# Linear attention on one core: the state product as four 64x64 parts, key sums on GpSimd, and a new order of the unit's work

## The chip, the cores and the metric

The kernel runs on one core of one Trainium2 chip. The metric is device time in microseconds (us) of one launch; less is better. Before the change it is 872.39 us (median of 3 runs, 872.06 to 872.72).

## What is computed

Three layers follow one another: linear attention, a feed-forward layer with a mixing over tokens, and a mixture of experts. The change touches the first one alone. Its reference, for batch 4, 8 heads, sequence 576, head dimension 64 and 128 features:

```
def phi(x):
    proj = np.einsum('bhsd,df->bhsf', x, w_phi)
    proj = proj - np.max(np.abs(proj), axis=-1, keepdims=True)
    return np.concatenate([np.exp(proj), np.exp(-proj)], axis=-1)
q_p, k_p = (phi(q), phi(k))
kv = np.einsum('bhsf,bhsd->bhfd', k_p, v)
z = np.sum(k_p, axis=2)
num = np.einsum('bhsf,bhfd->bhsd', q_p, kv)
den = np.einsum('bhsf,bhf->bhs', q_p, z)[..., None] + 1e-06
return (num / den).astype(np.float32)
```

`kv` is the state, `z` are the key sums. Afterwards `u = x + (x.T @ U @ V).T` (the mixing, with factors U and V of rank 32), a hidden layer of 2048, and the experts.

## The kernel before

**Units.** Two (batch, head) pairs make a unit; partitions 0 to 63 hold one pair, 64 to 127 the other ("halves"). There are 16 units of 9 token tiles of 64 rows (T = 9). The attention is a pipeline of 18 steps: in step s, PE (TensorE) works on the newest unit s (transposes of raw q and k, `transposes`), on the newer unit s-1 (projection by w_phi, `project`) and on the older unit s-2 (the turned queries `turn_q`, the state product `state`, the output product `output`). Steps 0 to 3 and 16, 17 are written out, steps 4 to 15 run in a loop of two steps. Every engine has its own in-order list of work; semaphores join them.

**The engines of one step.** DVE (VectorE) reads each projection from PSUM twice, for the greatest absolute value (L1014) and to subtract it (L1022), in three groups per unit, and divides the output of an earlier unit (`divide`, L1030 to L1037). ACT (ScalarE) copies the transposed q and k out of PSUM (`evac_T`, L840), makes exp(x) and exp(-x) of the turned queries (`exp_q`, L845, L846) and of the keys (`exp_k`, L853, L854), and copies the finished state out (`evac_kv`, L861). The work on transposes, turned queries and keys is cut in three groups of three tiles (NG, GT).

**The state product before.** For each of the 9 tiles, each sign of the exponent and each half, one matmul (L1533) has 128 features of `kp` as its stationary operand and 65 columns of `vv` moving: 64 of v and a column of ones, which gives the key sum with the state. The 36 matmuls of a unit are spread over the step between transposes and turns, cut by the constant LATE. The state comes out with features on partitions, which is how the output product (L1549) wants it.

**GpSimd before.** POOL splits the weights of the feed-forward layer into a high and a low part (`split_piece`, L677 and L680), one piece for two steps of attention, as they arrive by DMA. When the pieces of the first matrix are done, it makes the factor V ready in both parts (`spread_v`, L716 to L728), and raises the semaphore uv_ready up to 8. Behind that it waits for the last output product (n_done) and splits the second matrix.

**The end of the attention.** In step 16 PE has, behind the output product of unit 14, the product of the rows by U (job "odd", L1671, 18 matmuls of 64 rows by 64 columns with 512 moving columns). In step 17 it has, ahead of the output product of unit 15, the three "mix" jobs of the first block (L1685, L1686), which read what `spread_v` makes:

```
                    if c == 0:
                        pe.wait_ge(uv_ready, 8)
```

Then come the transposes "uT" of the first block and the feed-forward layer.

## Time and profile before

| | us |
|---|---|
| median of 3 runs | 872.39 |
| the profiled execution's own time | 872.83 |
| its span | 870.7 |
| PE busy | 857.1 |
| DVE busy | 402.4 |
| ACT busy | 342.1 |
| POOL busy | 153.6 |

The span is the time from the first to the last instruction in the trace; the execution's own time is 2.1 us longer. Busy time of PE counts records of matmuls, which overlap in its pipeline, so that it says when PE had work and not how well it was used. A matmul in fp32 leaves two records in the trace: "x72" are 36 matmuls. A start in the timeline, less the start of the row ahead of it on the same engine, is what that row's work took of the engine.

### The profile page before, as it was taken

How to read it: one execution, taken by the hardware profiler on the slowest of the kernel's cores; microseconds unless marked ns; L12 is line 12 of the kernel's file. 1: busy time of each engine (PE TensorE's matmuls, PEld its weight loads, DVE VectorE, ACT ScalarE, POOL GpSimd, SP SyncE). 2: the span in 40 equal slices, each digit the busy share in tenths (PEclk: the TensorE clock that was granted, in tenths of full speed). 3: DMA queues.
4: the chain of work that ended last, by engine and by line, in shares of the span. 5: the costliest groups of instructions: out<-in, count | busy, mean ns of one | idle time of the engine just before them, and what ended most of it. 6: DMA issues, size and time to landing. Idle time of an engine off the chain costs nothing.

```text
span 870.7 us, 19055 instructions
## 1 busy us (share of the span) xinstructions
PE 857.1 (98%) x6984; PEld 749.7 (86%) x6985; DVE 402.4 (46%) x732; ACT 342.1 (39%) x767; POOL 153.6 (18%) x158
## 2 busy tenths in 40 slices
PE   7999999999999999999999999999999999999996
PEld 6999999789899899799989889998778888888885
DVE  4676776531245335425635663552773342432221
ACT  3677666521136326414612531541332342432221
POOL 0311222476000000000000000029152121212111
PEclk9999999999999999999999999999999999999999
DMA  6644442227522102102101210513431341311111
GB/s 139 160 116 126 130 117 78 65 92 55 1 73 61 37 37 61 49 0 71 63 13 49 59 39 37 193 49 134 156 127 69 134 148 36 126 48 42 36 36 42
DMA packets 52469, 67.65 MB, mean 78 GB/s; under 512 B 29768, under 2 KB 29896, under 8 KB 52424
## 3 DMA queue, kind: packets, MB, share of 16 engines
q1 hardware_dynamic: 42552, 44.90, 19.7%
q10 hardware_dynamic: 6512, 11.64, 4.4%
q0 software_dynamic: 3360, 10.49, 3.7%
q8 instruction: 31, 0.51, 0.3%
q14 instruction: 14, 0.11, 0.0%
HBM read 57.58 MB, written 9.98 MB: 78 GB/s over the span
## 4 chain that ended last, share of the span: by engine, by line
PE 93%; DVE 3%; ACT 1%; issue 1%; DMA 0%; POOLq 0%; SPq 0%; DVEq 0%; ACTq 0%
PE bank L1619 23%; PE bank L1621 23%; PE bank L1620 23%; PE bank L1533 8%; PE bank L1549 4%; PE bank L1506 4%; PE bank L1808 2%; PE bank L1494 1%; PE bank L1517 1%; PE bank L1671 1%; PE bank L1760 1%; PE bank L1690 1%; DVE stage L1094 1%; ACT stage L916 1%; PE bank L1685 1%
## 5 line engine op out<-in xcount | busy, mean ns | idle before, releaser
L1063 DVE SCALAR_TENSOR_TENSOR hid_lo<-bank,hid_hi 128x384 fp32r<-128x384 f32 x96 | 53.5, 558 | 211.1 <-ACT hid_hi L892 211.1
L1619 PE MATMUL bank<-uT_hi,W 128*128 128x384 f32 x384 | 129.4, 337 | 0.3 <-DVE uT_lo L1082 0.3
L1621 PE MATMUL bank<-uT_hi,W 128*128 128x384 f32 x384 | 129.6, 337 | 0.0
L1620 PE MATMUL bank<-uT_lo,W 128*128 128x384 f32 x384 | 128.9, 336 | 0.0
L892 ACT ACTIVATE hid_hi<-bank 128x384 fp32r<-128x384 f32 x96 | 46.9, 488 | 185.5 <-PE bank L1621 185.3
L916 ACT ACTIVATE stage<-stage 128x512 f32<-128x512 f32 x135 | 84.6, 627 | 78.6 <-DVE stage L1094 72.1
L1619 PE MATMUL bank<-W,hid_hi 128*128 128x512 f32 x288 | 114.1, 396 | 0.7 <-DVE hid_lo L1063 0.7
L1621 PE MATMUL bank<-W,hid_lo 128*128 128x512 f32 x288 | 113.7, 395 | 0.0
L1620 PE MATMUL bank<-W,hid_hi 128*128 128x512 f32 x288 | 113.4, 394 | 0.0
L1094 DVE TENSOR_TENSOR stage<-rows,stage 128x512 f32<-128x512 f32 x135 | 89.0, 687 | 9.8 <-ACT stage L916 8.5
L1325 DVE TENSOR_TENSOR hT_lo<-bank,hT_hi 128x512 fp32r<-128x512 f32 x40 | 27.7, 691 | 105.5 <-ACT hT_hi L953 105.5
L1619 PEld LDWEIGHTS bank<-uT_hi,W 128*128 128x128 f32 x384 | 72.2, 188 | 4.3 <-DVE uT_lo L1082 0.5
L1533 PE MATMUL bank<-vv,kp 64*128 64x65 f32 x1152 | 75.3, 273 | 0.0
L1620 PEld LDWEIGHTS bank<-uT_lo,W 128*128 128x128 f32 x384 | 72.1, 188 | 3.8
L947 ACT ACTIVATE hrow<-bank 128x512 f32<-128x512 f32 x40 | 23.9, 599 | 125.7 <-PE bank L1621 125.7
L1621 PEld LDWEIGHTS bank<-uT_hi,W 128*128 128x128 f32 x384 | 72.0, 188 | 0.0
L1533 PEld LDWEIGHTS bank<-vv,kp 64*128 64x128 f32 x1152 | 69.8, 188 | 2.0 <-issue 0.8
L1619 PE MATMUL bank<-W,xT_hi 128*128 (+1 forms) x160 | 64.9, 405 | 0.3 <-DVE xT_lo L1320 0.2
L1619 PEld LDWEIGHTS bank<-W,hid_hi 128*128 128x128 f32 x288 | 54.1, 188 | 12.7 <-issue 1.8
L1619 PE MATMUL bank<-W,hT_hi 128*128 (+1 forms) x160 | 64.2, 401 | 0.0
L1621 PEld LDWEIGHTS bank<-W,hid_lo 128*128 128x128 f32 x288 | 54.0, 188 | 11.7
L1014 DVE TENSOR_REDUCE top<-bank 128x6 f32<-128x768 f32 x48 | 45.7, 952 | 37.3 <-PE bank L1506 37.3
(274 smaller groups left out, 1430.4 us busy)
## 6 DMA issues: line engine op xcount, KB each, us to landing
rows<-in_moe_w SPq DMA_DIRECT2D x12, 1024.0 KB, 6.4
stage<-gate_rows ACTq DMA_DIRECT2D x38, 256.0 KB, 3.2
stage<-in_moe_w_ch SPq DMA_DIRECT2D x16, 512.0 KB, 3.9
qk_raw<-in_q SPq DMA_DIRECT2D x32, 144.0 KB, 2.9
vv<-in_v SPq DMA_DIRECT2D x32, 144.0 KB, 3.2
x_rows<-rows SPq DMA_DIRECT2D x6, 768.0 KB, 3.2
qk_raw<-in_k SPq DMA_DIRECT2D x30, 144.0 KB, 2.9
late_stage<-in_moe_w SPq DMA_DIRECT2D x4, 1024.0 KB, 6.0
```

The source lines that it names most:

```text
L892: act.activation(hid_hi[:, n % 2], bank[:, HB[n % 2], 0:TOK], ACT.Relu).then_inc(hid_hi_out, 1)
L916: act.activation(product(m), product(m), ACT.Copy, accum_out=logits[:, b * BLK + i, g:g + 1])\
L1014: dve.tensor_reduce(most, src, AX.X, ALU.max, apply_absolute_value=True).then_inc(top_done, 1)
L1063: dve.scalar_tensor_tensor(out=hid_lo[:, n % 2], in0=bank[:, HB[n % 2], 0:TOK], scalar=0.0, in1=hid_hi[:, n % 2].bitcast(F32), op0=ALU.max ...
L1094: dve.tensor_tensor(product(m), rows[:, b * BLK + i, :], gate_row(k), ALU.mult)\
L1325: dve.tensor_tensor(hT_lo[:, 4 * g:4 * g + 4], bank[:, 2 + g, :].rearrange("p (c n) -> p c n", c=4), hT_hi[:, 4 * g:4 * g + 4].bitcast(F32 ...
L1506: mm = pe.matmul(bank[:, pair + a, t * NF:t * NF + NF], qkT[rr, g, t, :], wphi[rr, :], start=True, stop=True)
L1533: mm = pe.matmul(bank[:, KV_BANK + half, sign * VW:(sign + 1) * VW], kp[par][rr, t // GT, t % GT, sign, :], vv[par][rr, t, :], start=(t == ...
L1549: mm = pe.matmul(dst[rr, t, :], qpT[:, n // GT, sign, n % GT, rr], kv[:, half, VW * sign:VW * sign + VW], start=(sign == 0), stop=(sign == 1))
L1619: pe.matmul(dst, lhs_hi, rhs_hi, start=start, stop=False)
L1620: pe.matmul(dst, lhs_hi, rhs_lo, start=False, stop=False)
L1621: return pe.matmul(dst, lhs_lo, rhs_hi, start=False, stop=stop)
```

## The change

- **State product.** `vv` becomes the stationary operand (64 rows, 64 columns) and `kp` the moving one (128 columns). The two signs go to the two halves of the output partitions, the two halves of the rows to two PSUM banks: four products on four quarters of the array. All 36 matmuls stand in one piece. The state now comes out with the features along the free dimension, and has no key sums.
- **Turning back.** `evac_kv_raw` copies the state to SBUF, `turn_kv` transposes it with four matmuls, and `evac_kv` copies it out again, now in two instructions.
- **Key sums.** `sum_keys` on POOL adds the nine tiles of `kp` in four additions: two of 768 elements per partition and two of 256. Four matmuls of one moving column (in `turn_kv`) then add over the partitions.
- **Groups.** Raw q and k are transposed in two groups, of 4 and 5 pairs of tiles, and the queries turned in two, of 5 and 4 tiles; projection and key exponentials stay in three.
- **Order.** PE and ACT have a new order within a step; on ACT the three `exp_k` of a unit now stand together at the end of the step. On POOL `sum_keys` stands ahead of each piece of weights, and ahead of `spread_v`.
- The column of ones in `vv`, and its two memsets on DVE, go.

The diff, cut:

```diff
+    TT = (4, T - 4)
+    NT = len(TT)
     OT = (5, T - 5)
...
+        K_TURNED = slice(NF, NF + 2 * D)
+        K_SUMS = slice(NF + 2 * D, NF + 2 * D + 2)
...
+            def sum_keys(u, par):
+                if not (isinstance(u, int) and u == 0):
+                    pool.wait_ge(k_summed, u)
+                pool.wait_ge(kp_done, NG * u + 2)
+                settled(pool)
+                pool.tensor_tensor(k_part[:, :, :, :], kp[par][:, 0], kp[par][:, 1], ALU.add).then_inc(k_step, 1)
+                pool.wait_ge(k_step, NG * u + 1)
+                pool.wait_ge(kp_done, NG * u + 3)
+                settled(pool)
+                pool.tensor_tensor(k_part[:, :, :, :], k_part[:, :, :, :], kp[par][:, 2], ALU.add).then_inc(k_step, 1)
+                pool.wait_ge(k_step, NG * u + 2)
+                settled(pool)
+                pool.tensor_tensor(k_part[:, 0], k_part[:, 0], k_part[:, 1], ALU.add).then_inc(k_step, 1)
+                pool.wait_ge(k_step, NG * u + 3)
+                if not (isinstance(u, int) and u < 2):
+                    pool.wait_ge(kv_turned, u - 1)
+                settled(pool)
+                pool.tensor_tensor(k_sum[par][:, :, :], k_part[:, 0], k_part[:, 2], ALU.add).then_inc(k_summed, 1)
...
             with pool.Fori(1, UNITS // 4) as n:
                 for i in range(2):
+                    sum_keys(4 * n + 2 * i, 0)
+                    sum_keys(4 * n + 2 * i + 1, 1)
                     split_piece(2 * n + i, i, 0, (2 * n + i) * WCH)
             spread_v()
...
                 def exp_k(u, p, g):
                     act.wait_ge(p_out, NG * u + (2, 3, 3)[g])
                     if not (isinstance(u, int) and u < 2):
                         act.wait_ge(kv_done, u - 1)
+                        act.wait_ge(k_summed, u - 1)
...
+                def evac_kv_raw():
+                    act.wait_ge(kv_done, s - 1)
+                    act.activation(kv_raw[:, :, :], bank[:, KV_BANK:KV_BANK + 2, 0:NF], ACT.Copy).then_inc(kv_raw_out, 1)
+
                 def evac_kv():
                     u = s - 2
-                    act.wait_ge(kv_done, u + 1)
+                    act.wait_ge(kv_turned, u + 1)
                     if not (isinstance(u, int) and u == 0):
                         act.wait_ge(n_done, OUTS * u)
-                    act.activation(kv[:, :, :], bank[:, KV_BANK:KV_BANK + 2, 0:2 * VW], ACT.Copy)\
-                       .then_inc(kv_out, 1)
+                    act.activation(kv.rearrange("p h s n -> p s h n")[:, :, :, 0:D],
+                                   bank[:, KV_BANK:KV_BANK + 2, K_TURNED].rearrange("p s (h n) -> p s h n", n=D), ACT.Copy)
+                    act.activation(kv[:, :, :, D], bank[:, KV_BANK:KV_BANK + 2, K_SUMS], ACT.Copy).then_inc(kv_out, 1)
...
+                def state():
                     u = s - 2
+                    pe.wait_ge(v_loaded[par], 32 * (u // 2) + 32)
+                    if not (isinstance(u, int) and u == 0):
+                        pe.wait_ge(n_out, OUTS * u)
+                    for t in range(T):
+                        if t in (0, 2 * GT):
+                            pe.wait_ge(kp_done, NG * u + 2 + t // (2 * GT))
+                            settled(pe)
+                        for sign, cols in enumerate(HALVES):
+                            for half, rr in enumerate(HALVES):
+                                mm = pe.matmul(bank[cols, KV_BANK + half, 0:NF], vv[par][rr, t, :],
+                                               kp[par][rr, t // GT, t % GT, sign, :], start=(t == 0), stop=(t == T - 1))
+                    mm.then_inc(kv_done, 1)
+
+                def turn_kv():
+                    u = s - 2
+                    pe.wait_ge(kv_raw_out, u + 1)
+                    settled(pe)
+                    for half in range(2):
+                        for sign, rr in enumerate(HALVES):
+                            pe.transpose(bank[:, KV_BANK + sign, NF + D * half:NF + D * half + D], kv_raw[rr, half, :],
+                                         ident[rr, rr])
+                    pe.wait_ge(k_summed, u + 1)
+                    settled(pe)
+                    for sign in range(2):
                         for half, rr in enumerate(HALVES):
+                            mm = pe.matmul(bank[:, KV_BANK + half, K_SUMS.start + sign:K_SUMS.start + sign + 1],
+                                           k_sum[par][rr, sign, :], ones[rr, 0:1], start=True, stop=True)
+                    mm.then_inc(kv_turned, 1)
```

**Where PE's work moved.** PE, one full step (step 3) before. The names: `qk_raw` raw q and k, `proj` projected queries being turned, `kp` with `vv` the state, `kv` with `qpT` the output.

```order
L1494 MATMUL bank<-ident,qk_raw 128x64 x6
L1506 MATMUL bank<-wphi,qkT 128x128 x12
L1517 MATMUL bank<-ident,proj 128x64 x6
L1533 MATMUL bank<-vv,kp 128x65 x12
L1494 MATMUL bank<-ident,qk_raw 128x64 x6
L1533 MATMUL bank<-vv,kp 128x65 x10
L1517 MATMUL bank<-ident,proj 128x64 x6
L1533 MATMUL bank<-vv,kp 128x65 x12
L1494 MATMUL bank<-ident,qk_raw 128x64 x6
L1533 MATMUL bank<-vv,kp 128x65 x2
L1506 MATMUL bank<-wphi,qkT 128x128 x6
L1517 MATMUL bank<-ident,proj 128x64 x6
```

PE, the same step of the change, with the output product that ends it (before, too, 36 of them ended the step).

```order
L1550 MATMUL bank<-ident,proj 128x64 x10
L1540 MATMUL bank<-wphi,qkT 128x128 x12
L1528 MATMUL bank<-ident,qk_raw 128x64 x8
L1565 MATMUL bank<-kp,vv 64x128 x36
L1550 MATMUL bank<-ident,proj 128x64 x8
L1540 MATMUL bank<-wphi,qkT 128x128 x6
L1575 MATMUL bank<-ident,kv_raw 128x64 x4
L1581 MATMUL bank<-ones,k_sum 128x1 x4
L1528 MATMUL bank<-ident,qk_raw 128x64 x10
L1595 MATMUL bank<-kv,qpT 64x65 x36
```

The state is one piece of 36 in place of four, six groups of transposes are four, and turning the state back and the key sums stand between the last projection and the output.

**Where GpSimd's work moved.** POOL, from the end of the loop over the pieces of the first matrix, before:

```order
L677 COPY W<-stage 128x1024
L678 REGISTER_ALU
L680 ISA
L680 TENSOR_TENSOR W<-stage,W 128x1024
L734 REGISTER_ALU
L734 COMPARE_AND_BRANCH
L716 MEMSET v_pair 128x1152
L721 COPY v_pair<-v_raw 32x9x64 x4
L724 CAST v_hl<-v_pair 128x1152
L728 TENSOR_TENSOR v_hl<-v_pair,v_hl 32x1152 x2
```

POOL in the change, from the last half of that loop's body (in its last round: the additions of unit 15, the last piece) to the same place:

```order
L749 TENSOR_TENSOR k_part<-kp 128x768
L750 REGISTER_ALU
L751 REGISTER_ALU
L753 TENSOR_TENSOR k_part<-k_part,kp 128x768
L756 TENSOR_TENSOR k_part<-k_part 128x256
L761 TENSOR_TENSOR k_sum<-k_part 128x256
L686 ISA
L689 ISA
L689 COPY W<-stage 128x1024
L690 REGISTER_ALU
L692 ISA
L692 TENSOR_TENSOR W<-stage,W 128x1024
L767 REGISTER_ALU
L767 COMPARE_AND_BRANCH
L728 MEMSET v_pair 128x1152
```

Four additions per unit now stand ahead of the pieces, and the work of `spread_v`, in its old place behind the loop, stands behind the additions of the last unit.

**ACT in one step of the change:** queries, transposes, the raw state, queries, the turned state, transposes, and then all keys of the newer unit.

```order
L881 ACTIVATE qpT<-bank 128x640
L882 ACTIVATE qpT<-bank 128x640
L875 ACTIVATE qkT<-bank 128x512
L895 ACTIVATE kv_raw<-bank 128x256
L881 ACTIVATE qpT<-bank 128x512
L882 ACTIVATE qpT<-bank 128x512
L902 ACTIVATE kv<-bank 128x2x2x64
L904 ACTIVATE kv<-bank 128x4
L875 ACTIVATE qkT<-bank 128x640
L890 ACTIVATE kp<-proj 128x3x128
L891 ACTIVATE kp<-proj 128x3x128
```

Before, the first group of keys stood at the end of a step, and the other two at the head of the next one, around a copy of transposes.

## Rows read from the trace of the kernel before

**Rows 1.** Page, part 1 (busy time) and part 4 (shares of the chain).

```profile
PE 857.1 (98%) x6984; PEld 749.7 (86%) x6985; DVE 402.4 (46%) x732; ACT 342.1 (39%) x767; POOL 153.6 (18%) x158
PE 93%; DVE 3%; ACT 1%; issue 1%; DMA 0%; POOLq 0%; SPq 0%; DVEq 0%; ACTq 0%
```

**Rows 2.** Busy time by stretch: attention (stretch, length, busy PE, PEld, DVE, ACT, POOL, clock, DMA).

```profile
98.10:157.80 59.70, 59.70 (x1318) 58.38 (x1316) 42.16 (x69) 41.20 (x97) 17.01 (x12) 1.00 0.41 109
```

**Rows 3.** Timeline of PE, one step (start, us, engine, line).

```profile
102.92 2.32 PE L1549 MATMUL bank<-kv,qpT 128*64 128x65 f32 x72
105.17 0.40 PE L1494 MATMUL bank<-ident,qk_raw 64*128 64x64 f32 x6
105.41 1.56 PE L1506 MATMUL bank<-wphi,qkT 64*128 64x128 f32 x24
106.80 0.34 PE L1517 MATMUL bank<-ident,proj 64*128 64x64 f32 x6
107.11 1.56 PE L1533 MATMUL bank<-vv,kp 64*128 64x65 f32 x24
108.50 0.35 PE L1494 MATMUL bank<-ident,qk_raw 64*128 64x64 f32 x6
108.69 1.28 PE L1533 MATMUL bank<-vv,kp 64*128 64x65 f32 x20
...
112.47 0.34 PE L1517 MATMUL bank<-ident,proj 64*128 64x64 f32 x6
112.74 2.32 PE L1549 MATMUL bank<-kv,qpT 128*64 128x65 f32 x72
```

**Rows 4.** Timeline of PE at the end of attention (steps 16 and 17).

```profile
161.28 2.32 PE L1549 MATMUL bank<-kv,qpT 128*64 128x65 f32 x72
163.53 4.51 PE L1671 MATMUL bank<-rows,u_pair 64*64 64x512 f32 x36
167.97 0.40 PE L1517 MATMUL bank<-ident,proj 64*128 64x64 f32 x6
...
169.64 1.08 PE L1678 MATMUL bank<-z_odd,ident 128*64 128x512 f32 x4
170.65 1.33 PE L1533 MATMUL bank<-vv,kp 64*128 64x65 f32 x20
...
174.35 0.50 PE L1685 MATMUL bank<-z_hi,v_hl 128*128 128x512 f32 x1
```

**Rows 5.** Timeline of ACT behind an output product's start.

```profile
103.79 0.53 ACT L853 ACTIVATE kp<-proj 128x384 f32<-128x384 f32 x1
104.20 0.53 ACT L854 ACTIVATE kp<-proj 128x384 f32<-128x384 f32 x1
```

**Rows 6.** Group of instructions of ACT (busy, mean ns, idle before).

```profile
L947 ACT ACTIVATE hrow<-bank 128x512 f32<-128x512 f32 x40 | 23.9, 599 | 125.7 <-PE bank L1621 125.7
```

**Rows 7.** Groups of instructions of POOL.

```profile
L680 POOL TENSOR_TENSOR W<-stage,W 128x1024 fp32r<-128x1024 f32 x10 | 24.0, 2398 | 1.8 <-POOL W L677 1.8
L680 POOL TENSOR_TENSOR W<-stage,W 128x1024 f32 x6 | 14.1, 2356 | 1.6 <-POOL W L677 1.6
L785 POOL TENSOR_TENSOR W<-rows,W 128x2048 fp32r<-128x2048 f32 x3 | 13.8, 4615 | 0.2
```

**Rows 8.** Timeline of POOL, the last piece and the preparation of V.

```profile
148.30 2.35 POOL L680 TENSOR_TENSOR W<-stage,W 128x1024 f32 x1 [0.26 <-POOL W L677]
150.59 1.06 POOL L716 MEMSET v_pair<- 128x1152 f32 x1
...
158.12 5.34 POOL L728 TENSOR_TENSOR v_hl<-v_pair,v_hl 32x1152 fp32r<-32x1152 f32 x2
```

**Rows 9.** Stretches at the end of the span (same columns as rows 2).

```profile
867.00:870.70 3.70, 0.00 (x0) 0.00 (x0) 0.00 (x0) 0.00 (x0) 0.00 (x0) 0.55 0.09 36
```

**Rows 10.** Timeline of PE near the start, projection early and a little later.

```profile
8.07 1.60 PE L1506 MATMUL bank<-wphi,qkT 64*128 64x128 f32 x12
12.13 0.91 PE L1506 MATMUL bank<-wphi,qkT 64*128 64x128 f32 x12
```

More of the change, by code:

```diff
@@ L876, in step @@
                 if older:
+                    evac_kv_raw()
+                    if is_step(s, UNITS + 1):
+                        side(first_jobs[1], 1)
                     exp_q(1)
+                    evac_kv()
                 if newest:
                     evac_T(s, 1)
-                if older:
-                    evac_kv()
-                    exp_q(2)
                 if newer:
-                    exp_k(s - 1, 1 - par, 0)
+                    for g in range(NG):
+                        exp_k(s - 1, 1 - par, g)
             def hidden(b, f):
@@ L998, in _ @@
         def _(dve):
-            for i in range(2):
-                dve.memset(vv[i][:, :, D:VW], 1.0).then_inc(v_padded, 1)
             dve.memset(ones[:, :], 1.0)
@@ L1490, in transposes @@
                     settled(pe)
-                    for t in range(GT):
-                        n = 2 * (g * GT + t)
+                    for t in range(TT[g]):
+                        n = 2 * (tiles_of(TT, g).start + t)
                         for half, rr in enumerate(HALVES):
@@ L1511, in turn_q @@
                     u = s - 2
[L1512 to L1513 removed]
+                    pe.wait_ge(p_out, NG * u + g + 1)
                     settled(pe)
[L1515 removed]
+                    for t in range(OT[g]):
                         for half, rr in enumerate(HALVES):
                             mm = pe.transpose(bank[:, TURN_BANK + half, t * HALF:t * HALF + HALF],
[L1518 removed]
+                                              proj[par][rr, OT[0] * g + t, :], ident[rr, rr])
@@ L1519, in turn_q @@
                     mm.then_inc(qt_done, 1)
-                def state(g, first=0, last=2 * T // NG):
+                def state():
                     u = s - 2
-                    if g < 2:
-                        pe.wait_ge(kp_done, NG * u + NG - 1 + g)
-                    if g == 0:
-                        pe.wait_ge(v_loaded[par], 32 * (u // 2) + 32)
-                        if not (isinstance(u, int) and u == 0):
-                            pe.wait_ge(n_out, OUTS * u)
-                    for n in range(2 * T // NG * g + first, 2 * T // NG * g + last):
-                        sign, t = n // T, n % T
-                        for half, rr in enumerate(HALVES):
-                            mm = pe.matmul(bank[:, KV_BANK + half, sign * VW:(sign + 1) * VW],
-                                           kp[par][rr, t // GT, t % GT, sign, :], vv[par][rr, t, :],
-                                           start=(t == 0), stop=(t == T - 1))
-                    if n == 2 * T - 1:
-                        mm.then_inc(kv_done, 1)
+                    pe.wait_ge(v_loaded[par], 32 * (u // 2) + 32)
[10 more added lines that the diff above has]
+                    mm.then_inc(kv_done, 1)
@@ L1555, in step @@
                         pe.wait_ge(const_loaded, 32)
-                        project(0)
-                    if isinstance(s, int) and s < 3:
-                        pe.wait_ge(t_out, NG * (s - 1) + 2)
-                    else:
-                        pe.wait_ge(qp_done, NG * (s - 2))
-                    transposes(s - 1, 1 - par, 2)
-                    if not is_first(s - 1):
-                        project(0)
-                if newer:
-                    project(1)
-                if older:
-                    if is_step(s, 2):
-                        keep_busy(4, 2)
-                    pe.wait_ge(t_out, NG * s if newer else NG * UNITS)
-                    turn_q(0)
-                    state(0)
-                    if is_step(s, UNITS + 1):
-                        side(first_jobs[1], 1)
+                    project(0)
+                    project(1)
                 if newest:
```

112 lines of the change are left out of this document (57 added, 55 removed).

## The prediction

> **What bounds the kernel now.** The page's busy times and its chain of waits come first: PE is busy for 98% of the span and holds 93% of the chain [rows 1]. In the attention stage PE is never idle, while DVE is busy for 42.16 of 59.70 us, ACT for 41.20 and POOL for 17.01 [rows 2]. So the timeline of PE is next. One step goes from output product to output product, 102.92 to 112.74, 9.82 us [rows 3]. 14 such steps lie between the output products of units 0 and 14. Last, the end of the attention, where jobs of the next layer are mixed in [rows 4], and POOL's own timeline beside it [rows 8].
>
> Why does the state product take so much? 24 of its records take 1.39 us, .058 each [rows 3], though they move 65 columns only. The projection moves 128 columns and takes .058 as well (24 in 1.39, 105.41 to 106.80). What both have in common is a stationary operand of 128 columns. Output products load 64 columns and take 2.25/72 = .031 per record. All three run two abreast. So the state pays for its weight loads, 72 x .056 = 4.03 us of every step.
>
> **The change part by part (per step).**
>
> *State product.* The kernel already has one product on four quarters of the array, the U job: 36 records of 512 columns in 4.44 us, .123 each, while the z job, two abreast, takes 1.01/4 = .252 for the same 512 [rows 4]. Four abreast halves it. For 128 columns the record two abreast is .058, so four abreast .029; loads of 64 columns are seen at .031. I take 72 x .029 = 2.1 us and .1 for a change of shape on either side, less what the four old pieces paid: **2.2 against 4.1 us**, a gain of 1.9. Upper bound, if the quarters ran two abreast: 72 x .058 = 4.2.
>
> The Trainium skill (TensorEngine Tiling (Array Packing), Key Properties) says that changing the tiling mode drains the engine; the step of .1 us between shapes is how I read it here, and by that rule nothing more is to be added.
>
> *Turns and transposes.* 36 matmuls before and after. Three pairs took .19 (108.50 to 108.69), mostly .06 per pair. Four groups in place of six: 1.25 against 1.4.
>
> *Turning back and key sums on PE.* Two pairs of transposes, .12; four matmuls with 128 columns of weights, 8 records at .056 and some latency, .5; together .65.
>
> PE alone would then have 2.25 (output) + 2.1 (projections, 18 x .116) + 1.25 + 2.2 + .65 = **8.5 us**. That would gain 1.3 per step, if PE never waited.
>
> *ACT.* An exp of 384 elements takes .53, and the next starts .41 to .42 later [rows 5]; 512 elements take .599 [rows 6], so 640 about .70. Per step: keys 6 x .42 = 2.5, queries 2 x .60 + 2 x .49 = 2.2, transposes .49 + .58, raw state .28, turned state .28 + .10. Sum 6.4 us of issue time, less than PE's. It does not bind by its sum but by its order, below.
>
> *POOL.* An addition of 1024 elements takes 2.356 us, one of 2048 4.615 [rows 7]: 2.2 ns per element and .1 us. So 768 take 1.79 and 256 take .66. A dependent instruction starts .26 later in the loop (the idle time in the first row) [rows 8]. The four additions are a chain: 1.79 + .26 + 1.79 + .26 + .66 + .26 + .66 = **5.7 us**. With half a piece of weights (1.8) POOL has 7.5 us per step. That fits, but each unit's chain lies on a path.
>
> The Trainium skill (GPSIMD Engine Reference, Performance versus the Vector engine) holds that elementwise work belongs on VectorE, about twice as fast, and gives 4.5 us for 2048 elements; the trace's 4.6 agrees. The move leaves DVE's load alone.
>
> *The loop of waits.* The keys now all stand behind `evac_kv` and the last copy of transposes in ACT's order, and `evac_kv` waits for the key sums. So one unit's keys wait for the unit before: copy of transposes .58; four exps, after which POOL may start, 1.68; semaphores .2; POOL 5.7; semaphore .1; key sum matmuls .5 and .2 until they land; `evac_kv` .28 and .10. Sum **9.3 us**, and that is a cycle: a step can't be shorter, whatever PE has to do. PE fills 8.5 of it and waits at three places for ACT or POOL. A second cycle, through ACT and PE without POOL (exp of queries, transposes, state, raw state, exp, turned state) comes by the same numbers to 9.2. I take 9.3. Over 14 steps: 14 x (9.82 - 9.3) = **-7.3 us**.
>
> *Start.* The first output product has the longer way (raw state, turning, key sums of unit 0 in series, and all its keys after the third projection) ahead of it once: **+1.2**, by the terms above (.38 + .12 + .7, with the keys' delay partly hidden). Bounds 0 and 3.
>
> *DMA and SP.* The same loads; `next_unit` waits for 2 groups in place of 3, whose end lies about as late in the step. POOL's pieces come up to 3 us later, with a full period of two steps to spare. Nothing. DVE loses its memsets before any work: nothing.
>
> *End of the attention.* This is the term that I think decides. Before, POOL was done with the pieces early; `spread_v` runs from 150.59 to 163.46 (158.12 + 5.34), 12.87 us [rows 8], and the first mix job at 174.35 [rows 4] finds it ready 11 us ahead. Now `spread_v` stands behind the additions of unit 15 and the last piece. From the start of the output product of unit 14: keys of unit 15, 2.0 us until POOL may start; additions 5.7; piece 3.6; `spread_v` 12.9. The mix job can start at **24.2**. Before, it was 174.35 - 161.28 = 13.07. PE meanwhile has output 2.25, U job 4.44, turn .4, state 2.2, z 1.0, turn .3, turning back .7: about 11.3, and stands still for some 12.9 us. Cost: 24.2 - 13.1 = **+11.1**. The last output product and the transposes stand behind the mix jobs; n_done behind the output; the split of the second matrix behind n_done: all of it shifts as one.
>
> *Clock.* PE idle at the end of the span has a mean granted clock of .55 [rows 9], so the level falls from 2.4 to 1.2 GHz when PE stands still. Projection of 12 records near the start took 1.60 us, and .91 shortly after [rows 10], a factor of 1.8. About 6 us of work (mix, output, transposes) follow the standstill; at half rate throughout they would cost 5 more, if the level came back at once nothing. I take **+2.5**, ends 0 and 6.
>
> The Trainium skill (TensorE: Matmul & The Clock Gate, Why this matters for your kernels) asks for no idle gaps between bursts, else half rate; the row agrees.
>
> **Sum** against the profiled execution: 872.83 - 7.3 + 1.2 + 11.1 + 2.5 = 880.3 us, span 878.2. That execution stands .4 above the median of the runs, so I give **880.0**.
>
> **Rivals.**
>
> *A. PE-bound steps: not slower.* If the chain is shorter than I think (waits of .26 nearer .1, additions faster), PE would set the step. At 8.5 us: 14 x 1.32 = 18.5 gained, 872.8 - 18.5 + 1.2 + 11.1 + 2.5 = 869. The point from which it decides is 8.76 per step, where 14 x 1.06 equals the 14.8 lost at both ends. For it: PE's sum is small. Against it: both cycles come out above 9, and only the exps and additions, measured, make 7.4 of 9.3. Chance .13.
>
> *B. POOL's additions are slower.* POOL and DVE may hinder each other. At 15% more per element, the chain is .7 longer, the step 10.0, and the time 872.8 + 2.5 + 1.2 + 11.8 + 2.5 = 891. Against it: 2.356 us during attention, where DVE is busy, and 2.398 after it [rows 7]; but operands there were loads, not what ACT has just written. Chance .12. The Trainium skill (GPSIMD Engine Reference, Specifications) tells of shared ports when DVE has two inputs in SBUF; the rows show no such slowing.
>
> *C. The four parts run two abreast.* State 4.2, in series with the chain at ACT: step about 11.2, 872.8 + 19 + 1 + 11 + 2.5 = 906. Against it: .123 against .252 in the U job. It had other operands and 512 columns. Chance .05.
>
> *D. The end costs nothing*, since `spread_v` is hidden in some way I overlook: 880 - 13.6 = 866. The order on POOL and the wait for 8 speak against it. Chance .04.
>
> My forecast has the rest, .66.
>
> **How the numbers follow.** The forecast's own range: step 9.1 to 9.6 (-2.8 to +4.2), clock and start (-3.7 to +5): some 875 to 887. To leave out no more than 2 in 10, I go down toward A, whose cases between 8.6 and 9.0 give 870 to 876, and up toward B: 872 to 891. Slower by over .2% (1.7 us, about what a measurement of this kernel can tell from no change) is the forecast, B and C: .66 + .12 + .05 = .83, less .02 for its lower edge, .81. Faster: D and most of A, .13. Same: .06.
>
> **What would show it.** In the profile after: records of the state product at .029 with starts in fours; a step of 9.3 from output to output; PE waiting before the output product for ACT's `kv`, and POOL's four additions starting at once behind the second group of keys; then PE idle for about 13 us ahead of L1718, POOL busy all that time with `spread_v`, and a granted clock below 1 behind it. It is wrong if that gap is under 5 us, if steps are under 8.8 or over 9.7, or if the state takes over 3 us.

## The result, and the profile after

The change makes the kernel slower: **883.88 us** (median of 4 runs, 882.14 to 887.85) against 872.56 for the kernel before on the same chip (4 runs, 872.06 to 872.78), a ratio of 1.0137 with a 95% interval of 1.0101 to 1.0173. The profiled execution took 882.14 us, its span is 880.1, against 872.83 and 870.7.

Page of the changed kernel, parts 1 and 4:

```profile
PE 845.7 (96%) x7176; PEld 730.8 (83%) x7177; DVE 403.7 (46%) x730; ACT 341.4 (39%) x751; POOL 234.4 (27%) x222
PE 87%; ACT 4%; DVE 3%; POOL 3%; issue 3%; ACTq 0%; POOLq 0%; DVEq 0%
```

PE has 11.4 us less to do than before [rows 1] and the kernel is 9.4 longer, so PE stands still in places where it did not before. Where, is read in three stretches.

**One step in the steady part.** PE's timeline of the changed kernel:

```profile
103.16 2.32 PE L1595 MATMUL bank<-kv,qpT 128*64 128x65 f32 x72 [0.17 <-ACT kv L904]
105.41 0.52 PE L1550 MATMUL bank<-ident,proj 64*128 64x64 f32 x10
105.77 1.55 PE L1540 MATMUL bank<-wphi,qkT 64*128 64x128 f32 x24
107.48 0.46 PE L1528 MATMUL bank<-ident,qk_raw 64*128 64x64 f32 x8 [0.16 <-issue]
107.98 2.19 PE L1565 MATMUL bank<-kp,vv 64*64 64x128 f32 x72
110.10 0.47 PE L1550 MATMUL bank<-ident,proj 64*128 64x64 f32 x8
110.41 0.89 PE L1540 MATMUL bank<-wphi,qkT 64*128 64x128 f32 x12
111.13 0.28 PE L1575 MATMUL bank<-ident,kv_raw 64*128 64x64 f32 x4
111.42 0.61 PE L1581 MATMUL bank<-ones,k_sum 64*128 64x1 f32 x8
111.86 0.54 PE L1528 MATMUL bank<-ident,qk_raw 64*128 64x64 f32 x10
112.57 2.32 PE L1595 MATMUL bank<-kv,qpT 128*64 128x65 f32 x72 [0.18 <-ACT kv L904]
```

From output to output it is 9.41 us, against 9.82 [rows 3]. The state product is one row: 107.98 to 110.10, 2.12 us for 72 records, .029 each. PE now has small holes ahead of the transposes and of the output; what it waits for there is ACT (like rows ahead of the transposes in other steps name ACT's exps, and some, as this one, issue). One more wait is printed nowhere: the key sums start .29 behind the four turns of the state (111.13 to 111.42), which take .12 where nothing is waited for (22.69 to 22.81 in the same kernel). ACT and then POOL in the same step:

```profile
102.93 0.17 ACT L904 ACTIVATE kv<-bank 128x4 f32<-128x4 f32 x1
103.02 0.70 ACT L875 ACTIVATE qkT<-bank 128x640 f32<-128x640 f32 x1
...
104.86 0.51 ACT L891 ACTIVATE kp<-proj 128x384 f32<-128x384 f32 x1
...
112.07 0.39 ACT L902 ACTIVATE kv<-bank 128x256 f32<-128x256 f32 x1 [0.37 <-PE bank L1581]
```

```profile
105.55 1.82 POOL L749 TENSOR_TENSOR k_part<-kp 128x768 f32<-128x768 f32 x1 [3.69 <-ACT kp L891]
107.62 1.82 POOL L753 TENSOR_TENSOR k_part<-k_part,kp 128x768 f32<-128x768 f32 x1 [0.25 <-POOL k_part L749]
109.61 0.72 POOL L756 TENSOR_TENSOR k_part<-k_part 128x256 f32<-128x256 f32 x1 [0.18 <-POOL k_part L753]
110.54 0.73 POOL L761 TENSOR_TENSOR k_sum<-k_part 128x256 f32<-128x256 f32 x1 [0.20 <-POOL k_part L756]
```

The loop of waits that the prediction adds up can be walked here: copy of transposes at 103.02, four exps to 105.37, POOL 105.55 to 111.27 (5.72), key sums on PE at 111.42, the turned state at 112.07 and 112.35, next copy 112.43. That is one period of 9.41, and no link of it has room: the key sums start .15 behind the end of POOL's last addition. Whether this loop *alone* sets the period, these rows can't say: everything in a steady loop repeats with the same period.

**The end of the attention.** PE (with the output product of unit 14 first), then POOL:

```profile
159.70 2.32 PE L1595 MATMUL bank<-kv,qpT 128*64 128x65 f32 x72 [0.54 <-ACT kv L904]
161.95 4.51 PE L1704 MATMUL bank<-rows,u_pair 64*64 64x512 f32 x36
...
170.40 0.56 PE L1581 MATMUL bank<-ones,k_sum 64*128 64x1 f32 x8
183.50 0.76 PE L1718 MATMUL bank<-z_hi,v_hl 128*128 128x512 f32 x1 [12.54 <-POOL v_hl L740]
...
186.62 2.32 PE L1595 MATMUL bank<-kv,qpT 128*64 128x65 f32 x72
```

```profile
166.44 0.73 POOL L761 TENSOR_TENSOR k_sum<-k_part 128x256 f32<-128x256 f32 x1 [0.20 <-POOL k_part L756]
...
170.71 1.06 POOL L728 MEMSET v_pair<- 128x1152 f32 x1
171.83 4.95 POOL L733 COPY v_pair<-v_raw 32x576 f32<-32x576 f32 x4
...
178.07 5.28 POOL L740 TENSOR_TENSOR v_hl<-v_pair,v_hl 32x1152 fp32r<-32x1152 f32 x2
```

PE has nothing for 12.54 us while POOL works with gaps of .3 us at most. The first mix job starts 23.80 behind the output product of unit 14; before it was 13.07 [rows 4]. The granted clock falls to .5 at 173.0, in this gap, and is whole again at 186.6. By stretch (columns as in rows 2):

```profile
170.00:184.00 14.00, 1.46 (x23) 1.37 (x22) 0.69 (x1) 1.92 (x5) 12.88 (x9) 0.61 0.12 37
184.00:188.00 4.00, 4.00 (x52) 2.54 (x52) 2.08 (x3) 0.00 (x0) 0.00 (x0) 0.67 0.00 0
```

**The start.** PE at the first output product:

```profile
23.92 2.32 PE L1595 MATMUL bank<-kv,qpT 128*64 128x65 f32 x72
...
26.53 0.89 PE L1540 MATMUL bank<-wphi,qkT 64*128 64x128 f32 x12
29.51 1.40 PE L1540 MATMUL bank<-wphi,qkT 64*128 64x128 f32 x11 [2.10 <-issue]
```

In the middle of a projection PE stops for 2.10 us and the trace names nobody that it waits for. Right behind, the granted clock is .5 for 3.4 us.

The whole difference, cut at the starts of output products (kernel before: first at 24.14, second at 33.78, that of unit 14 at 161.28, mix at 174.35, first feed-forward product at 180.57; after: 23.92, 36.58, 159.70, 183.50, 190.66):

| | before | after | difference | forecast |
|---|---|---|---|---|
| to the first output | 24.14 | 23.92 | -0.22 | +1.2 |
| step from unit 0 to 1 | 9.64 | 12.66 | +3.02 | -0.5 |
| 13 further steps | 127.50 | 123.12 | -4.38 | -6.8 |
| output of unit 14 to mix | 13.07 | 23.80 | +10.73 | +11.1 |
| mix to feed-forward | 6.22 | 7.16 | +0.94 | +2.5 (clock) |
| the rest | 690.1 | 689.4 | -0.7 | 0 |
| span | 870.7 | 880.1 | +9.4 | +7.5 |

### The profile page after: what moved, and what is told of

Same layout as the page of the kernel before. It is cut to its first block, busy times and chain, and to the rows that moved or that the text cites. A ratio compares the mean times of both kernels' runs of the same rounds, so it can differ in the third digit from the quotient of the medians.

```text
span 880.1 us, 19643 instructions
## 1 busy us (share of the span) xinstructions
PE 845.7 (96%) x7176; PEld 730.8 (83%) x7177; DVE 403.7 (46%) x730; ACT 341.4 (39%) x751; POOL 234.4 (27%) x222
## 3 DMA queue, kind: packets, MB, share of 16 engines
HBM read 57.58 MB, written 9.98 MB: 77 GB/s over the span
## 4 chain that ended last, share of the span: by engine, by line
PE 87%; ACT 4%; DVE 3%; POOL 3%; issue 3%; ACTq 0%; POOLq 0%; DVEq 0%
PE bank L1652 23%; PE bank L1654 23%; PE bank L1653 22%; PE bank L1565 4%; PE bank L1540 3%; PE bank L1841 2%; PE bank L1595 2%; PE bank L1528 1%; PE bank L1550 1%; PE bank L1793 1%; PE bank L1581 1%; ACT kp L890 1%; PE bank L1723 1%; PE bank L1509 1%; DVE stage L1128 1%
## 5 line engine op out<-in xcount | busy, mean ns | idle before, releaser
L1652 PE MATMUL bank<-W,hT_hi 128*128 (+1 forms) x160 | 64.4, 403 | 0.0
L1654 PE MATMUL bank<-W,hT_lo 128*128 (+1 forms) x160 | 62.7, 392 | 0.0
L1653 PE MATMUL bank<-W,hT_hi 128*128 (+1 forms) x160 | 62.5, 391 | 0.0
L1654 PE MATMUL bank<-W,xT_lo 128*128 (+1 forms) x160 | 62.5, 391 | 0.0
```

Of the source, the lines that this page charges most:

```text
L1652: pe.matmul(dst, lhs_hi, rhs_hi, start=start, stop=False)
L1653: pe.matmul(dst, lhs_hi, rhs_lo, start=False, stop=False)
L1654: return pe.matmul(dst, lhs_lo, rhs_hi, start=False, stop=stop)
```

## The experiments

Theory 1 for the slowdown: the preparation of V behind the last additions costs all of it (some 12 us with the clock), and steps gain .4 each. Theory 2 for the size of that gain: the loop of waits through POOL's additions sets the step. Its rival: the second cycle, through ACT and PE alone. (In the expectations of extra_add and fewer_add the loop through POOL is called theory 1; from fewer_keys on theory 2 is the second cycle.)

**no_v: nothing left to wait for at the end.** On the changed kernel; V's preparation is replaced by zeros made ahead of all additions, which leaves out the mixing's result and keeps PE's work.

```diff
+            for n in range(7):
+                pool.memset(v_pair[:, n:n + 3, :], 0.0).then_inc(uv_ready, 1)
...
-            spread_v()
```

Expected:

> The changed kernel without the preparation of V behind the loop: the factor V is replaced by zeros, made by GpSimd before its first addition (the mixing adds nothing then). Theory 1 (PE stands still at the end of attention for V alone): the 12.5 us gap of PE ahead of the first mix job goes to under 1 us, the granted clock stays at 1.00 there, and the time falls by 10.7 + 0.9 of the change, plus up to 1 more: 871 to 873 us, about equal to the kernel before. Rival (something else is late there too, say the last piece of weights or the key sums of unit 15): a gap of 3 us or more stays, 875 or more. In both the steps stay at 9.41 us, and the long step behind unit 0 may stay.

Measured: 871.58 us (median of 10), ratio to the kernel before .9997 (.9977 to 1.0016).

```profile
160.37 2.32 PE L1599 MATMUL bank<-kv,qpT 128*64 128x65 f32 x72 [0.54 <-ACT kv L908]
...
172.26 0.48 PE L1722 MATMUL bank<-z_hi,v_hl 128*128 128x512 f32 x1 [0.63 <-DVE z_lo L1113]
```

The gap of 12.54 is .63, and the mix job starts 11.89 behind the output. So V's place costs the changed kernel about 12.3 us (883.88 - 871.58). Without it the kernel is no faster than before, though: the pause at the start is still here (second step 12.67).

**early_v: the same, with all the work done.** V is loaded right behind the first q, placed before the additions of unit 0 and split behind them.

```diff
+            for n in range(4):
+                sp.dma_start(v_raw[RANK * n:RANK * n + RANK, :], V).then_inc(vraw_loaded, 16)
             load_qk(1, 1)
...
+            place_v()
             for u in range(4):
                 sum_keys(u, u % 2)
+                if u == 0:
+                    split_v()
...
-            spread_v()
```

Expected:

> The changed kernel with V loaded right behind the first q and prepared by GpSimd in two parts, one before the additions of unit 0 and one behind them. Nothing is left out. Theory 1: the gap goes as in no_v, and GpSimd is idle in those places (1.45 to 15.3 us and 20.9 to 26.5 us), so the time is that of no_v, 871 to 874 us. Rival (the early part makes the key sums of units 0 and 1 late, or the loads hinder those of q and k): the first output product starts 1 to 4 us later than 23.92, 874 to 877 us.

Measured: 870.4 us (10 runs), ratio .9976 (.9958 to .9994). Moving 12.9 us of POOL's work brings back 13.5. These are not V's place alone: in the traces the stretch from the output product of unit 14 to the mix job is 10.3 us shorter (13.47 for 23.80) and the second step 3.05, while the first output comes 1.25 later.

```profile
157.90 3.89 PE L1600 MATMUL bank<-kv,qpT 128*64 128x65 f32 x72 [0.54 <-ACT kv L909]
...
171.37 0.47 PE L1723 MATMUL bank<-z_hi,v_hl 128*128 128x512 f32 x1 [0.63 <-DVE z_lo L1114]
```

Here the step from unit 0 to 1 is 9.61, without a pause. New is that the output product of unit 14 takes 3.82 in place of 2.25: ahead of it PE waited .75 and .54 us, and the granted clock is .5 from 158.0 to 161.4. All kernels that follow stand on this one.

**extra_add: a fifth addition on POOL.** An addition of 256 elements more in each unit's chain, of data that nobody reads.

```diff
+                pool.tensor_tensor(k_part[:, 1], k_part[:, 1], k_part[:, 1], ALU.add)
```

Expected:

> early_v with one more addition of 256 elements on GpSimd ahead of the last one of each unit (its result is not used). It puts 0.7 us more into the chain from keys to key sums. Theory 1 (the step is the cycle through GpSimd, measured 9.41): each step grows by 0.7, to 10.1 us. Rival (PE and ACT set the step and GpSimd is just in time): 0 to 0.3 us more. About 14 x 0.7 = 9.8 us more in all by theory 1.

Measured: 877.11 us (one run), steps of 9.98, .57 more. PE's rows now name POOL; POOL's own stand below:

```profile
113.71 0.28 PE L1581 MATMUL bank<-ident,kv_raw 64*128 64x64 f32 x4
114.57 0.61 PE L1587 MATMUL bank<-ones,k_sum 64*128 64x1 f32 x8 [0.58 <-POOL k_sum L765]
```

```profile
108.13 1.82 POOL L752 TENSOR_TENSOR k_part<-kp 128x768 f32<-128x768 f32 x1 [3.69 <-ACT kp L897]
...
113.13 0.61 POOL L764 TENSOR_TENSOR k_part<-k_part 128x256 f32<-128x256 f32 x1 [0.20 <-POOL k_part L759]
113.70 0.73 POOL L765 TENSOR_TENSOR k_sum<-k_part 128x256 f32<-128x256 f32 x1
```

The last addition follows the new one at once, so that this one costs .57 from start to start. The chain takes 6.30 us (108.13 to 114.43) in place of 5.72: .58 more, and all of it arrives in the step. So POOL's chain had nothing to spare at 9.41 (.01 at most): its cycle **does bind** there, as theory 2 says.

**fewer_add: the third addition left out.** The key sums then lack a third of the tiles.

```diff
-                pool.tensor_tensor(k_part[:, 0], k_part[:, 0], k_part[:, 1], ALU.add).then_inc(k_step, 1)
```

Expected:

> early_v without the third addition of the key sums (the key sums lack one third of the tiles then). 0.92 us less in the chain. Theory 1 with the second cycle through ACT and PE close behind it (9.2 by my working): steps of 9.2 us, 0.2 shorter. Rival A (the cycle through GpSimd is the only one above PE's own work): 8.5 to 8.6 us. Rival B (GpSimd is not in the cycle): 9.41 unchanged.

Measured: 871.9 us (one run). The chain is .9 shorter and the step still 9.41, as from one group of transposes to its like. PE, then ACT:

```profile
105.41 0.52 PE L1531 MATMUL bank<-ident,qk_raw 64*128 64x64 f32 x10
...
110.43 0.47 PE L1531 MATMUL bank<-ident,qk_raw 64*128 64x64 f32 x8 [0.33 <-issue]
110.96 2.20 PE L1568 MATMUL bank<-kp,vv 64*64 64x128 f32 x72
...
114.11 0.28 PE L1578 MATMUL bank<-ident,kv_raw 64*128 64x64 f32 x4
114.23 0.56 PE L1584 MATMUL bank<-ones,k_sum 64*128 64x1 f32 x8
114.82 0.53 PE L1531 MATMUL bank<-ident,qk_raw 64*128 64x64 f32 x10
```

```profile
105.97 0.70 ACT L878 ACTIVATE qkT<-bank 128x640 f32<-128x640 f32 x1
106.57 0.52 ACT L893 ACTIVATE kp<-proj 128x384 f32<-128x384 f32 x1
...
109.05 0.68 ACT L884 ACTIVATE qpT<-bank 128x640 f32<-128x640 f32 x1
...
113.21 0.38 ACT L898 ACTIVATE kv_raw<-bank 128x256 f32<-128x256 f32 x1 [1.68 <-PE bank L1568]
```

By its number this is the rival that has GpSimd outside the cycle, but extra_add rules that out. What both show together: **two cycles have the same length**. Without the third addition the key sums wait for POOL no more (.12 behind the turns of the state, in place of .29), and the other cycle holds the step. It can be read off here. Second transposes 105.41, their copy 105.97, six exps of keys 106.57 to 109.05, two of queries until PE's first transposes at 110.43 (they need the bank that those exps read), state product 110.96, raw state 113.21, two exps of queries, second transposes 114.82: .56 + .60 + 2.48 + 1.38 + .53 + 2.25 + .38 + 1.23 = 9.41. How near the two are in the changed kernel: there the last exp of queries ends at 111.69; with the .14 that lie here between its end (114.68) and the transposes, those could have started at 111.83, and behind the key sums they start at 111.86. (The pause at the start is 2.52 us here, and that step 14.42.)

**fewer_keys: shorten the rival cycle.** As fewer_add, and the exp(-k) of the third group is left out (its place holds ones), which takes one activation out of ACT's order.

```diff
+                    if g < 2:
+                        act.activation(kp[p][:, g, :, 1, :], src, ACT.Exp, scale=-1.0).then_inc(kp_done, 1)
```

Expected:

> fewer_add (third addition left out) without the second exponential of the third group of keys, which ScalarE makes last before the first exponentials of the queries (exp(-k) is 1 there for three tiles, set once). 0.41 us less on ScalarE in the cycle: copy of transposes, keys, queries, transposes, state, raw state, queries, transposes. Theory 2 (with the third addition out, the step is that cycle, whose parts in the trace add up to 9.41): steps of 9.00 us. Rival (PE's own work and its changes of shape set 9.41): unchanged at 9.41.

Measured: steps of 9.08 to 9.21. With .41 of ACT's time taken away .2 to .3 of the step went; the rival, PE's own work, would have kept 9.41. So ACT's order is in the cycle that binds once the third addition is out. Part of what did not come is a stop of .13 on ACT ahead of the exps of queries (one starts at 110.76, .54 behind the last exp of keys, where .41 is the rule). The time as a whole, 896.55 us, says nothing of the step: what follows the first feed-forward product took 33 us longer than in fewer_add (171.26 to 894.5, against 179.85 to 869.8), probably since the experts get other tokens, which no row here shows.

**keys_split: the first group of keys ahead of the last copy of transposes.** All work is done.

```diff
+                if newer:
+                    exp_k(s - 1, 1 - par, 0)
                 if newest:
                     evac_T(s, 1)
                 if newer:
-                    for g in range(NG):
+                    for g in range(1, NG):
                         exp_k(s - 1, 1 - par, g)
```

Expected:

> early_v with the first group of keys ahead of the last copy of transposes on ScalarE, so that it fills the 0.17 us in which ScalarE waits for them. Everything behind in both cycles comes 0.17 earlier. Theory 2: steps of 9.24 us in place of 9.41 and 13 x 0.17 = 2.2 us less than early_v, 868 us. Rival (the turned queries' start waits for that copy, or the second group of keys for VectorE): 9.41 or more.

Measured: 869.61 us (10 runs), ratio .9961 (.9947 to .9976), faster than both kernels. Steps are 9.38, not 9.24. POOL's cycle stands in the way, and the trace shows it without room: state copied at 110.99, first keys 111.32, copy of transposes 112.15, second keys to 113.67, POOL 113.85 to 119.57, key sums 119.72, next state 120.36. Copy and keys only changed places in it. The wait of .17 that the expectation wanted to fill was not there in early_v either: its copy starts .09 behind the state's last part (110.55 to 110.64). The step from unit 0 to 1 is 12.53 again.

**two_sums: the third addition on PE.** Eight one-column matmuls in place of four; all work is done.

```diff
+                            pe.matmul(bank[:, KV_BANK + half, K_SUMS.start + sign:K_SUMS.start + sign + 1],
+                                      k_part[rr, 1, sign, :], ones[rr, 0:1], start=True, stop=False)
```

Expected:

> early_v with the third addition moved from GpSimd to PE: eight matmuls of one column in place of four add two tiles over the partitions. The chain on GpSimd is 0.92 shorter, PE has 0.45 us more between the turned state and the transposes. Theory 2 (PE's work in that place lies in the second cycle, because the transposes start right behind it): steps of 9.7 to 9.9 us. Rival (only ScalarE's end of the queries releases the transposes): 9.41 to 9.5 us.

Measured: 871.45 us (one run), steps 9.63 to 9.68. The key sums take .87 on PE in place of .44. Of these .43 more, .15 fall where the second transposes wait for ACT anyway (114.67 to 114.82 in fewer_add); the rest is what the step grew by, .22 to .27. PE has holes elsewhere and POOL got .9 back, and neither helps.

**late_w: is it the crowd of loads at the start?** In the changed kernel the DMA engines are 94% taken up from 24 to 28 us. Here the first pieces of weights and U wait for the second state product.

```diff
+            sp.wait_ge(kv_done, 2)
```

Expected:

> early_v with the loads of the first two pieces of weights and of U on the SyncE queue held back until the state of unit 1 is done (about 32 us in place of 22). Theory 3 (PE's pause of 2 us behind unit 0, ahead of whose end a packet of instructions of 16 KB moves among the loads, comes from the crowd of loads from 24 to 30 us): no pause in the profile in the step behind unit 0, and the ten-odd times of this kernel lie closer than those of early_v (869.2 to 873.7): within 1.5 us. Rival (the pause is chance or comes from something else): the same spread. The median 869 to 871 by both.

Measured: 872.07 us (10 runs), ratio .9997 (.9982 to 1.0012). The step has no pause, but neither has that of early_v. The next one takes 15.91:

```profile
43.39 0.72 PE L1534 MATMUL bank<-ident,qk_raw 64*128 64x64 f32 x8 [4.24 <-DMA qk_raw<-in_k]
44.20 4.12 PE L1571 MATMUL bank<-kp,vv 64*64 64x128 f32 x72
```

The moved loads are now ahead of the keys of unit 3 in SP's queue, and PE waits 4.24 us for those, then works at half clock. So the test of the crowd failed. The times don't lie closer either, as was expected (869.93 to 874.72, against 869.18 to 873.68 for early_v).

**thin_crowd: fewer loads, and none of them late.** On keys_split, which has the pause; the second piece of weights goes behind q and k of unit 4, U behind those of unit 5.

```diff
+            sp.dma_start(stage[:, 0, :], w_ch1_rows[:, 0, 0:WCH]).then_inc(wst_loaded[0], 16)
+            next_unit(4, 0)
+            sp.dma_start(stage[:, 1, :], w_ch1_rows[:, 0, WCH:2 * WCH]).then_inc(wst_loaded[1], 16)
+            next_unit(5, 1)
```

Expected:

> Against keys_split: of the loads that are issued together from 21.6 to 28.7 us, only V of unit 1 and the first piece of weights stay; the second piece goes out behind q and k of unit 4, and the four loads of U (whose issues take 4.84 us) behind those of unit 5. Theory (PE's pause of 2 us in the step from unit 0 to unit 1 hangs on the crowd of loads at 22 to 29 us; keys_split took 12.53 for that step): the step takes 9.5 to 9.9, PE has no pause ahead of a projection near 28 us and the clock stays whole, mix at 168.7 to 169.3, span 865 to 865.6, median about 866.8, provided that no later load is late. Rival (the pause comes from something else, as code for PE that arrives late or the place where the instructions lie): the step stays at 12 to 13 and the median at 869 to 870.

Measured: 869.26 us (10 runs), ratio .9965 (.9950 to .9979). PE waits for no load, the step is 12.27 and the pause is there:

```profile
30.29 1.12 PE L1555 MATMUL bank<-wphi,qkT 64*128 64x128 f32 x11 [1.70 <-issue]
```

It is shorter (1.70 for 1.96) but falls at the same place in PE's program, though the DMA engines are .81 taken up from 24 to 28 us in place of .96. The loads that were taken away are not the cause.

**moved_code: shift PE's program.** On keys_split; the same place in the program in six kernels suggests PE's instructions themselves, which come in packets of 16 KB in a DMA queue of their own. Twelve more stand ahead of everything.

```diff
-            keep_busy(4, 2)
+            for _ in range(16):
+                pe.matmul(bank[:, 7, 0:HALF], ident[:, :], ident[:, 0:HALF], start=True, stop=True)
```

Expected:

> Against keys_split: the 4 wide matmuls with which PE starts become 16 narrow ones, which adds 12 instructions to PE's program ahead of everything and leaves the rest as it is. Theory (PE's pause near 27 us is its program arriving late, at a fixed distance in the code): the pause of about 2 us, which keys_split has behind the first 6 matmuls of the projection in the step from unit 0 to unit 1, moves 12 matmuls ahead: those 6 and 6 of the 10 turns of queries stand behind it, so 4 of the turns (4 records for the first 8, about x4) come before the pause. The step stays at 12 to 13. Rival (the pause hangs on a moment in time, on loads or on another engine): it stays behind 12 records of the projection, or near 27.2 us whatever stands there.

Measured: 871.19 us (one run). The pause is gone, which neither reading had foreseen (the step is 10.67 all the same; in it PE waits 1.11 us for POOL's key sums). But the 16 matmuls took 7.0 us in place of 3.8 and the first output came at 28.31 (keys_split: 23.71), so the packets also had more time.

**moved_8: shift it at no cost in time.** Both pieces of four wide matmuls (at the start, and ahead of the first state product) become eight of half the width.

```diff
-            keep_busy(4, 2)
+            keep_busy(8, 1)
```

Expected:

> Against keys_split: both pieces of 4 wide matmuls that keep PE busy (at its start, and ahead of the first state product) become 8 half as wide, the same columns, so 4 instructions more stand ahead of each. moved_code had 12 more at the start, lost PE's pause, and paid 4.6 us for its slow start (first output 28.31 against 23.71). Theory (the pause is PE's program arriving late, and where the packets' borders lie in it decides): with 8 instructions more and no time added, first output at 23.6 to 24.1, the step from unit 0 to unit 1 9.6 to 10.5 without a pause, span 865.3 to 866.5, median 867 to 868.5. Rival (moved_code lost the pause only because its start was later by 4.6 us, so that the packets had more time): the pause stays, step 12 to 13, median 869 to 870.

Measured: **868.09 us** (4 runs, 867.63 to 869.46), ratio .9948 (.9931 to .9965), the lowest median of this study; the interval of keys_split overlaps it.

```profile
33.74 0.77 PE L1547 MATMUL bank<-wphi,qkT 64*128 64x128 f32 x9
35.10 0.38 PE L1547 MATMUL bank<-wphi,qkT 64*128 64x128 f32 x2 [0.59 <-issue]
...
36.64 2.32 PE L1602 MATMUL bank<-kv,qpT 128*64 128x65 f32 x72 [0.17 <-ACT kv L909]
```

No pause in the old place and a step of 10.02, but a short stop of .59 one projection further on, and another of .68 at 51.37 (step 10.26). And the first output comes at 26.62, 2.9 us later than in keys_split: the granted clock is .5 from 14.4 to 21.3. So the second output is at 36.64 against 36.24, no earlier. The gain against keys_split shows in the span by .7 and lies inside the spread of that kernel's runs. The theory's first half held (no pause in the old place), its price did not. That these two always trade against each other is not shown: early_v has its second output at 34.78.

What all these traces have in common is the second 16 KB packet of that queue:

| | first output | packet starts | pause in this place | PE goes on, behind the packet's start |
|---|---|---|---|---|
| after | 23.92 | 27.08 | 2.10 | 2.43 |
| no_v | 24.00 | 27.24 | 2.10 | 2.35 |
| fewer_add | 25.12 | 28.77 | 2.52 | 2.37 |
| fewer_keys | 23.77 | 26.45 | 1.53 | 2.35 |
| keys_split | 23.71 | 26.93 | 1.96 | 2.24 |
| thin_crowd | 25.10 | 27.78 | 1.70 | 2.51 |
| before | 24.14 | 25.73 | none | |
| late_w | 25.37 | 25.94 | none | |
| extra_add | 25.63 | 26.18 | none | |
| early_v, two_sums, moved_code, moved_8 | 25.17 to 28.31 | 1.7 to 2.4 ahead of the output | none | |

Where the packet starts over 2.6 us behind the first output, PE stands still until 2.2 to 2.5 us after its start. Where it starts within 1.6 us or earlier, PE runs through there. Later stops agree: those of moved_8 end 2.83 and 2.55 us behind packets that start at 32.27 and 48.82, and one of .50 us in thin_crowd (42.61) ends 2.42 behind a packet at 40.19. All this fits PE's own program arriving late. It is argued and not shown: the traces don't say which engine's program a packet holds, and no run moved a packet alone. What makes the packet start early or late stays open. No change of the kernel's data loads moved it in a way that was foreseen.

## Why the prediction was right, and where it was not

The time on record was 880.0 with 872 to 891; it is 883.88. The sign and the main reason held, some terms were off in size (step, start and clock above all), and one was missing. By its steps:

- **State product, right.** 2.12 us against the 2.2 of the forecast. The U job's .123 against .252 in [rows 4] told it, and rival C with 906 is out.
- **Transposes and turns, too low.** The four groups take .36, .50 and .31 from start to start and the last .54 in busy time, some 1.7 with hand-overs in it, against 1.25. It enters PE's sum of 8.5 and not the 9.3.
- **Turning back, right.** From 111.13 to 111.86 it is .73, of which .17 is waiting for POOL: .56 against .65.
- **POOL's chain, right.** 5.72 against 5.7, with 1.82 and .72 for single additions (forecast 1.79 and .66) and shorter starts (.18 to .25 for .26). Rival B with slow additions did not come.
- **The step, right in kind and off in size.** "Sum **9.3 us**, and that is a cycle" names what binds: POOL's chain had nothing to spare (extra_add). The sum is .1 too low. It counts the four exps as 1.68, but POOL may start only when the fourth has ended, 1.75 behind the copy; and from the chain's end to the key sums it is .15, not .1. The second cycle, "by the same numbers to 9.2", was .2 too low: it is 9.41 too (fewer_add). Its raw state takes .38 of ACT (110.23 to 110.61), where the forecast's list has .28; what else was short can't be told, since the forecast gave that sum without its terms. The gain was .41 a step, not .52; over 13 steps 1.4 us. The rest of that row's gap, 1.0 us, is for the most part in the first three of them (9.74, 9.53, 9.59) and in what the 13 steps of before had saved against 9.82.
- **Start, too high.** -.2 for +1.2. Two of its parts lie beside other work: the raw state is copied at 21.80 while PE turns queries and projects (21.66 to 22.69), and POOL was done with the additions at 20.92. The number is one trace's: kernels with the same code on PE up to there have their first output from 23.71 (keys_split) to 25.63 (extra_add).
- **DMA and code, missed.** "The same loads ... Nothing" left out the pause: +3.5 against the forecast step, the largest single error. 2.10 of it are PE standing still and about .95 the half clock behind (early_v's step without it is 9.61).
- **End of the attention, right.** Mix job 23.8 behind the output product against 24.2, PE idle 12.54 against 12.9. no_v and early_v confirm the cause: 12.3 and 13.5 us come back, the latter with the pause. Rival D is out.
- **Clock, too dear.** +.94 against +2.5. The granted clock did fall, to .61 and .67 on average by stretch, but it was whole again at 186.6, when the three mix jobs were done (3.12 us against 2.15 in early_v, 171.37 to 173.52); the output product ran at full speed. The forecast had 6 us of work in the low state; it was 3.
- **Sum.** Against the forecast's span: start -1.4, pause +3.5, 13 steps +2.4, end -.4, clock -1.6, rest -.7, together 1.9 before rounding (880.1 against 878.2). That the total came so near is in part luck: 5.9 us of it were too little and 4.1 too much. That the median of runs stands 1.7 above the profiled one, no term tells.

Rival A, steps set by PE alone, did not come, and would not have come with a shorter chain on POOL either: fewer_add and fewer_keys come to 9.41 and 9.1 and not near 8.5. What the change had to win on PE, 1.3 us a step, came to a third, since PE, ACT and POOL hand each other a unit's parts in a fixed order.

## What to carry to other kernels

When work moves to an engine that "has room", look for what stands *behind* it in that engine's queue and who waits for that: here 5.7 us of additions per unit lie in a cycle no longer than the one through ACT and PE beside it, and 12.9 us of unrelated preparation behind the last of them cost 12 to 13. It comes back by moving that preparation to the front of the queue (early_v), and only then the new step is worth anything: 1.9 us, and 4 us with a better order of ACT and PE's start (moved_8 against the kernel before).

To learn which of two cycles sets a steady loop, lengthen one and shorten it, and read both answers together. A cycle that binds passes a longer piece on in full (.57 for .58). If a shorter one then gives nothing (0 for .9), another cycle of the same length stands beside it, and both have to be shortened. Read what a piece costs from start to start in the trace, and not from its duration: the added instruction shows .61 alone, the like of it .72, and the chain grew by .58.

## What the runs showed of the hardware that was not expected

- Four products on four quarters of the array run at .029 us a record of 128 fp32 columns, with 64x64 operands, 36 matmuls in 2.12 us; the price of changing shape behind them can't be told from zero in these rows (the next one, at 110.10, follows at once).
- PE can stop 1.5 to 2.5 us in the middle of a row of equal matmuls, with no engine or load that it waits for; the trace calls it issue. Six kernels of thirteen had it, at the same place of the code. That it waits for its own program is the reading that fits, and is not shown.
- Waits of .75 and .54 us, 1.2 us apart, were followed by 3.4 us at half clock in early_v; the same waits in no_v (.73 and .54) were not. Nine kernels have such a pair of waits there (.69 to 1.30, then .54): in early_v, extra_add, keys_split and thin_crowd the output product behind it takes 3.7 to 3.8 us, in the other five 2.25. What decides it is not known.
